# Gate logits made by token between output tiles, and a Sinkhorn iteration of five steps over five half groups

## The chip, the cores and the metric

The kernel runs on one core of a Trainium2 chip. The metric is the device time of one execution in microseconds (us), median of several runs. Before the change it is 1752.17 us (3 runs, 1752.05 to 1754.75).

## The reference

Three stages follow each other. All operands are float32.

```
p_packed = softmax(scale * p @ k.T) @ v            # 4 batches x 8 heads, 32 packed rows
a        = softmax(scale * q @ p_packed.T) @ p_packed   # 576 rows per batch and head
x        = a as [N = 2304 tokens, D = 512]
logits   = x @ w_gate                              # [N, E = 8]
P        = exp(logits - logits.max())              # one maximum over everything
8 times:  P /= P.sum(1) + 1e-9 ; P /= P.sum(0) + 1e-9 ; P *= N / E
x        = sum over e of P[:, e] * (relu(x @ w1[e]) @ w2[e])    # F = 1024
h        = relu(x @ w_in)                          # F = 2048
out      = (s * h * h + b) @ w_out
```

Each product of the experts and of the last stage is made of three passes over high and low parts (hi x hi, hi x lo, lo x hi), in a float32 type that TensorE runs in one pass.

## The kernel before, in words

The kernel is written by hand, one instruction stream per engine, with semaphores between them; nothing reorders it. TensorE (`pe`) multiplies, ScalarE (`act`) copies and exponentiates, VectorE (`dve`) makes the low parts, adds outputs and does the Sinkhorn steps, GpSimd (`pool`) splits weights and products into high and low parts, SyncE issues loads.

Since a is a product of the small attention weights `a` (here `a_hi`, `a_lo`, in the tensor `a_parts`: 2 quads of heads x 2304 tokens) and of the packed values, the kernel never forms x. It multiplies the packed values with the weights first (`packed_products`, `packed_gates`; results `g_parts` and, for the gate, `gw_both` and `gw_high`), and then with `a`.

The experts are 32 groups (8 experts x 4 parts of 256 hidden columns). A group has two half groups (u = 0, 1), each of 9 tiles of 128 tokens. A half group is written (g,u) below. On TensorE a half group is: four `hidden` calls (12 matmuls of 288 columns each; results in PSUM banks 2 to 5), between them two calls of `packed_products` for the next group, then nine output tiles (`outputs`, 6 matmuls of 512 columns each, PSUM banks 0 and 1 in turn). VectorE makes `h_lo` four times, then adds each output tile to `acc` (lines 1013 to 1021). Tile t on TensorE waits until VectorE has taken tile t-2. ScalarE makes `h_hi` and copies products to `g_raw`, which GpSimd splits (lines 557 and 559) as it does the weights (lines 534 to 551).

The gate: behind the outputs of half group (0,0), `gate_logits` makes logits by expert. The stationary side is `gw_both` (16 useful columns in 128: 8 of the high part, 8 of the low part, the rest zeros that GpSimd's memsets wrote) or `gw_high`, and the tokens move, 288 at a time: 8 spans x 2 quads x 2 = 32 matmuls. ScalarE copies each span (16 rows) to `logitsT`, which lies in the `acc` tensor. After two `hidden` calls, `turn_logits` turns it into tokens by expert with 18 transposes, and VectorE reads them (`logits_by_token`), finds the maximum, and the exponential follows in half group (1,0).

Sinkhorn: VectorE takes a step behind some of the output tiles (`sinkhorn`, line 1037). In each of the half groups (1,0), (1,1), (2,0), (2,1) two iterations are done, their steps behind tiles 0 to 4 and 5 to 8: sums and inverses of the rows, product by row, column part, column inverses (which needs a matmul with `ones` on TensorE behind the same tile, result in bank 7), product by column. The second iteration of a half group does its last two steps behind tile 8. Groups 1 to 3 add unscaled outputs; the finished gate is needed when `acc` is scaled, behind half group (3,1).

All matmuls have line 1221 (transposes have lines 1241, 1425 and 1455), the helper that records them, so they are told apart by tensors: `PS<-a_parts,gw_both` are the logits, `PS<-a_parts,g_parts` the hidden matmuls, `PS<-w_hi,h_hi` (and the two like it) the outputs, `PS<-w_hi,pp_parts` the packed products, `PS<-col_sum,ones` the column sums, which as float32 are two passes each.

Of the kernel before, what the change touches and what calls it, by code (L numbers as in the profile page):

```python
# [5 lines left out]
F32 = mybir.dt.float32  # L6
# [12 lines left out]
def attention_moe_mlp(nc, q, k, v, p, w_gate, w1, w2, w_in, w_out, s_, b_, out):  # L19
# [36 lines left out]
    with ExitStack() as ctx:  # L56
# [36 lines left out]
        gw_both = sb("gw_both", [P, QUADS, B, P], F32R)  # L93
        gw_high = sb("gw_high", [P, QUADS, B, P], F32R)
# [60 lines left out]
        logitsT = scratch[0:2 * E, UT * DM:UT * DM + N]  # L155
# [4 lines left out]
        LAST_TR, LAST_S2B = (5, 4, 3), (4, 6, 4)  # L160

        GWB, LG, LGT = 7, (2, 3, 4, 5), 0
# [29 lines left out]
        wg_ready = sem("wg_ready")  # L192
# [3 lines left out]
        lg_copied = sem("lg_copied")  # L196
        lgT_full = sem("lgT_full")
# [34 lines left out]
        SINKHORN_UNITS = [(1, 0), (1, 1), (2, 0), (2, 1)]  # L232
        COLUMN_SUMS = [(g, u, t) for g, u in SINKHORN_UNITS for t in (3, UT - 1)]
        assert len(COLUMN_SUMS) == SINKHORN_ITERATIONS
        UNSCALED = PER_EXPERT
        FIRST = UNSCALED + 1

# [284 lines left out]
        def _(pool):  # L522
# [4 lines left out]
            nc.gpsimd.memset(gw_both[:].bitcast(F32), 0.0).then_inc(wg_ready, 1)  # L527
            nc.gpsimd.memset(gw_high[:].bitcast(F32), 0.0).then_inc(wg_ready, 1)
# [86 lines left out]
        def _(act):  # L615
# [252 lines left out]
        def _(dve):  # L868
# [104 lines left out]
            def row_inverses():  # L973
                link(nc.vector.tensor_reduce(row_sum[:], gate[:], AX.X, ALU.add))
                link(nc.vector.tensor_scalar(row_sum[:], row_sum[:], EPS, None, ALU.add))
                link(nc.vector.reciprocal(row_inverse[:], row_sum[:]))  # L976

            def rows_divided():
                link(nc.vector.tensor_tensor(gate[:], gate[:], row_inverse[:].unsqueeze(2).to_broadcast([P, TILES, E]),  # L979
                                             ALU.mult))  # L980
# [737 lines left out]
```

## Time and profile before

| | before |
|---|---|
| median of 3 runs | 1752.17 us (1752.05 to 1754.75) |
| profiled execution | 1751.18 us |
| its span | 1749.4 us |
| PE (TensorE matmul) busy | 1739.2 us, 99% |
| PEld (TensorE weight load) busy | 1516.6 us, 87% |
| DVE (VectorE) busy | 916.5 us, 52% |
| ACT (ScalarE) busy | 710.0 us, 41% |
| POOL (GpSimd) busy | 609.1 us, 35% |

The span runs from the first to the last instruction; the time of an execution is 1.8 us more. Matmuls overlap: a listed duration holds the way through the array, so the pace of a stream is read from start to start. Busy time of an engine that is not waited for costs nothing.

### The profile page before, as it was taken

How to read it: one execution, taken by the hardware profiler on the slowest of the kernel's cores; microseconds unless marked ns; L12 is line 12 of the kernel's file. 1: busy time of each engine (PE TensorE's matmuls, PEld its weight loads, DVE VectorE, ACT ScalarE, POOL GpSimd, SP SyncE). 2: the span in 40 equal slices, each digit the busy share in tenths (PEclk: the TensorE clock that was granted, in tenths of full speed). 3: DMA queues.
4: the chain of work that ended last, by engine and by line, in shares of the span. 5: the costliest groups of instructions: out<-in, count | busy, mean ns of one | idle time of the engine just before them, and what ended most of it. 6: DMA issues, size and time to landing. Idle time of an engine off the chain costs nothing.

```text
span 1749.4 us, 27331 instructions
## 1 busy us (share of the span) xinstructions
PE 1739.2 (99%) x10257; PEld 1516.6 (87%) x10257; DVE 916.5 (52%) x1371; ACT 710.0 (41%) x1564; POOL 609.1 (35%) x380
## 2 busy tenths in 40 slices
PE   9999999999999999999999999999999999999999
PEld 7888888898889888888889888988888888888887
DVE  4846645445544445445544454455446555555555
ACT  5544465344434443444344443444343222222222
POOL 1263334434444344444444344344441001111100
PEclk9999999999999999999999999999999999999999
DMA  9431111111211111111211111112000000000002
GB/s 282 119 74 44 40 37 37 37 37 36 58 38 36 48 36 36 36 36 45 51 36 48 36 36 36 36 36 58 26 24 25 13 25 25 25 24 24 0 0 108
DMA packets 71776, 78.81 MB, mean 45 GB/s; under 512 B 7984, under 2 KB 59184, under 8 KB 71728
## 3 DMA queue, kind: packets, MB, share of 16 engines
q1 hardware_dynamic: 71728, 78.15, 16.6%
q8 instruction: 33, 0.54, 0.1%
q14 instruction: 15, 0.12, 0.0%
HBM read 73.42 MB, written 4.72 MB: 45 GB/s over the span
## 4 chain that ended last, share of the span: by engine, by line
PE 97%; DVE 1%; SPq 1%; DMA 0%; ACT 0%; issue 0%; DVEq 0%
PE PS L1221 95%; PE PS L1241 1%; DVE acc L1016 1%; DMA k_raw<-k_dram 0%; PE PS L1455 0%; DVE gate L993 0%; SPq L413 0%; ACT g_raw L617 0%; DVE gate L979 0%; SPq L437 0%; SPq L430 0%; SPq L418 0%; PE PS L1425 0%; DVE col_sum L983 0%; DVE row_inverse L976 0%
## 5 line engine op out<-in xcount | busy, mean ns | idle before, releaser
L1221 PE MATMUL PS<-w_hi,h_hi 128*128 128x512 f32 x1440 | 563.5, 391 | 1.3 <-DVE acc L1016 1.3
L1221 PE MATMUL PS<-w_hi,h_lo 128*128 128x512 f32 x1440 | 561.0, 390 | 0.0
L1221 PE MATMUL PS<-w_lo,h_hi 128*128 128x512 f32 x1440 | 560.8, 389 | 0.0
L1021 DVE SCALAR_TENSOR_TENSOR acc<-PS,gate,acc 128x512 f32<-128x512 f32 x504 | 377.8, 750 | 267.1 <-PE PS L1221 267.1
L694 ACT ACTIVATE h_hi<-PS 128x576 fp32r<-128x576 f32 x256 | 167.0, 653 | 675.1 <-PE PS L1221 674.4
L1221 PE MATMUL PS<-a_parts,g_parts 128*128 128x288 f32 x3072 | 438.1, 295 | 0.0
L1221 PEld LDWEIGHTS PS<-a_parts,g_parts 128*128 128x128 f32 x3072 | 419.3, 188 | 5.3 <-issue 0.4
L617 ACT ACTIVATE g_raw<-PS 32x256 f32<-32x256 f32 x992 | 373.1, 376 | 14.5 <-PE PS L1221 0.4
L1002 DVE SCALAR_TENSOR_TENSOR h_lo<-PS,h_hi 128x576 fp32r<-128x576 f32 x256 | 193.8, 757 | 323.5 <-ACT h_hi L694 323.4
L1221 PEld LDWEIGHTS PS<-w_hi,h_hi 128*128 128x128 f32 x1440 | 270.4, 188 | 57.7 <-DVE acc L1016 3.8
L1221 PEld LDWEIGHTS PS<-w_hi,h_lo 128*128 128x128 f32 x1440 | 270.3, 188 | 57.4
L1221 PEld LDWEIGHTS PS<-w_lo,h_hi 128*128 128x128 f32 x1440 | 270.4, 188 | 52.4
L534 POOL CAST w_hi<-stage 128x1024 fp32r<-128x1024 f32 (+1 forms) x78 | 76.8, 984 | 381.1 <-PE PS L1221 375.0
L557 POOL CAST g_parts<-g_raw 128x1024 fp32r<-128x1024 f32 x62 | 64.5, 1041 | 388.7 <-ACT g_raw L617 388.7
L536 POOL TENSOR_TENSOR w_lo<-stage,w_hi 128x1024 fp32r<-128x1024 f32 (+1 forms) x78 | 169.9, 2178 | 6.2
L1016 DVE TENSOR_TENSOR acc<-PS,acc 128x512 f32<-128x512 f32 x180 | 124.1, 689 | 54.1 <-PE PS L1221 53.4
L559 POOL TENSOR_TENSOR g_parts<-g_raw,g_parts 128x1024 fp32r<-128x1024 f32 x62 | 148.7, 2399 | 5.0
L852 ACT ACTIVATE mlp_f<-PS 128x512 f32<-128x512 f32 (+1 forms) x80 | 44.5, 556 | 220.0 <-PE PS L1221 220.0
L1221 PE MATMUL PS<-a_parts,w_hi 128*128 128x512 f32 (+1 forms) x320 | 117.8, 368 | 0.0
L1221 PE MATMUL PS<-a_parts,w_lo 128*128 128x512 f32 (+1 forms) x320 | 117.7, 368 | 0.0
L1221 PE MATMUL PS<-g_parts,w_hi 128*128 128x512 f32 (+1 forms) x320 | 117.7, 368 | 0.0
L1190 DVE SCALAR_TENSOR_TENSOR mlp_f<-mlp_f,s_and_b 128x512 f32<-128x512 f32 (+1 forms) x80 | 58.6, 733 | 100.4 <-ACT mlp_f L852 100.3
(131 smaller groups left out, 1051.8 us busy)
## 6 DMA issues: line engine op xcount, KB each, us to landing
stage<-moe_w_dram SPq DMA_DIRECT2D x96, 512.0 KB, 4.8
k_raw<-k_dram SPq DMA_DIRECT2D x8, 512.0 KB, 6.1
q_raw<-q_dram SPq DMA_DIRECT2D x8, 512.0 KB, 6.0
v_raw<-v_dram SPq DMA_DIRECT2D x8, 512.0 KB, 6.1
stage<-moe_w_in_dram SPq DMA_DIRECT2D x16, 256.0 KB, 2.8
stage<-moe_w_out_dram SPq DMA_DIRECT2D x8, 512.0 KB, 3.2
out_dram<-acc SPq DMA_DIRECT2D x16, 256.0 KB, 2.2
p_twice<-p_dram SPq DMA_DIRECT2D x8, 64.0 KB, 4.8
```

What stands on the lines that cost most here:

```text
L534: nc.gpsimd.tensor_copy(hi, src).then_inc(w1_ready, 1)
L536: nc.gpsimd.tensor_tensor(lo, src, hi.bitcast(F32), ALU.subtract).then_inc(w1_ready, 1)
L557: nc.gpsimd.tensor_copy(g_hi[par][:, Q], g_raw[Q][:]).then_inc(g_hi_ready, 1)
L559: nc.gpsimd.tensor_tensor(g_lo[par][:, Q], g_raw[Q][:], g_hi[par][:, Q].bitcast(F32), ALU.subtract).then_inc(g_lo_ready, 1)
L617: return nc.scalar.activation(dst, src, ACT.Copy)
L694: nc.scalar.activation(dst.rearrange("p (i n) -> p i n", i=2), src, ACT.Relu).then_inc(h_hi_ready, 1)
L852: nc.scalar.activation(mlp_f[:, slot, f, 0:n], bank(HB + 2 * slot + f, n), ACT.Relu).then_inc(relu_ready, 1)
L1002: nc.vector.scalar_tensor_tensor(out=h_lo[:, f, cols].rearrange("p (i n) -> p i n", i=2), in0=bank(HB + 2 * f, 2 * BANK).rearrange("p (i n ...
L1016: return nc.vector.tensor_tensor(dst, y, dst, ALU.add)
L1021: return nc.vector.scalar_tensor_tensor(out=dst, in0=y, scalar=share, in1=dst, op0=ALU.mult, op1=ALU.add)
L1190: nc.vector.scalar_tensor_tensor(out=r, in0=r, scalar=s_and_b[:, 0:1], in1=r, op0=ALU.mult, op1=ALU.mult).then_inc(f_ready, 1)
L1221: return nc.tensor.matmul(dst, lhsT, rhs, start=start, stop=stop)
```

## The change

There are two parts. Lines in the changed kernel are a few higher.

First, the logits are made by token. The tokens become the stationary side, 128 at a time, and `gw_both` (16 columns) or `gw_high` (8 columns) moves. The result of a tile of 128 tokens lands as [128 tokens, 16] in PSUM bank 5. A tile that lies in two batches (tiles 4 and 13) is done twice, with the gate of either batch, and VectorE takes the lower 64 rows from the second one. The matmuls stand between output tiles 4 to 8 of half group (0,0), three tiles of tokens (for tile 8: one) behind each output tile, and the last five tiles of tokens behind tile 8. The copies to `logitsT`, the transposes and the memsets are gone. The last transposes of the attention use bank 2 in place of 5, `hidden(0, 1, 0, 1)` waits until VectorE has read the logits, and a call of `packed_products` moves ahead of it.

Second, a Sinkhorn iteration is always five steps behind five successive tiles, and the eight iterations are spread over the half groups (1,0) to (3,0) by a list of starts. The reciprocal of the row sums moves from the first step to the second.

```
-        gw_both = sb("gw_both", [P, QUADS, B, P], F32R)
-        gw_high = sb("gw_high", [P, QUADS, B, P], F32R)
+        gw_both = sb("gw_both", [P, QUADS, B, 2 * E], F32R)
+        gw_high = sb("gw_high", [P, QUADS, B, 2 * E], F32R)
...
-        LAST_TR, LAST_S2B = (5, 4, 3), (4, 6, 4)
-        GWB, LG, LGT = 7, (2, 3, 4, 5), 0
+        LAST_TR, LAST_S2B = (2, 4, 3), (4, 6, 4)
+        GWB, LGB = 7, 5
+        HALVED = [t for t in range(TILES) if t * P // S != (t * P + P - 1) // S]
...
-        SINKHORN_UNITS = [(1, 0), (1, 1), (2, 0), (2, 1)]
-        COLUMN_SUMS = [(g, u, t) for g, u in SINKHORN_UNITS for t in (3, UT - 1)]
+        SINKHORN_UNITS = [(1, 0), (1, 1), (2, 0), (2, 1), (3, 0)]
+        SINKHORN_STARTS = [0, 5, 11, 17, 22, 27, 32, 37]
+        def sinkhorn_step(g, u, t):
+            if not isinstance(g, int) or (g, u) not in SINKHORN_UNITS:
+                return None
+            slot = SINKHORN_UNITS.index((g, u)) * UT + t
+            for i, first in enumerate(SINKHORN_STARTS):
+                if first <= slot < first + 5:
+                    return i, slot - first
+            return None
...
@ gpsimd
-            nc.gpsimd.memset(gw_both[:].bitcast(F32), 0.0).then_inc(wg_ready, 1)
-            nc.gpsimd.memset(gw_high[:].bitcast(F32), 0.0).then_inc(wg_ready, 1)
@ scalar
-            for n in range(2 * B):
-                act.wait_ge(lg_full, n + 1)
-                copy(logitsT[:, n * SPAN:(n + 1) * SPAN], bank(LG[n % 4], SPAN)[0:2 * E, :]
-                     ).then_inc(lg_copied, 1)
@ vector, logits_by_token
-                dve.wait_ge(lgT_full, 1)
-                by_token = bank(LGT)[:, 0:TILES * 2 * E].rearrange("p (t e) -> p t e", t=TILES)
+                dve.wait_ge(lg_full, 1)
+                both = bank(LGB)[:, 0:(TILES + len(HALVED)) * 2 * E].rearrange("p (t e) -> p t e", e=2 * E)
+                by_token, of_next = both[:, 0:TILES, :], both[HALF:P, TILES:TILES + len(HALVED), :]
                 link(nc.vector.tensor_copy(gate_part[:], by_token[:, :, E:2 * E]))
                 link(nc.vector.tensor_tensor(gate_part[:], by_token[:, :, 0:E], gate_part[:], ALU.add))
+                halves = gate_part[HALF:P, HALVED[0]:TILES:HALVED[1] - HALVED[0], :]
+                link(nc.vector.tensor_copy(halves, of_next[:, :, E:2 * E]))
+                link(nc.vector.tensor_tensor(halves, of_next[:, :, 0:E], halves, ALU.add))
@ vector, sinkhorn (steps 0 to 4 behind five successive tiles)
-                if t in (0, 5):
-                    row_inverses()
...
+                if step[1] == 0:
+                    row_sums()
+                if step[1] == 1:
+                    rows_divided()
+                if step[1] == 2:
+                    column_part()
+                if step[1] == 3:
+                    column_inverses(step[0])
+                if step[1] == 4:
+                    columns_divided(step[0])
@ vector: logits_by_token() moves ahead of lo_of_hidden(0, 1, 0, 0)
@ tensor
+            def gate_logits(tiles):
+                def tile(t, b, at):
+                    cols, cols_out = slice(t * P, (t + 1) * P), LGB * BANK + at * 2 * E
                     for Q in range(QUADS):
-                        mm(bank(LG[n % 4], SPAN), gw_both[:, Q, n // 2, :], a_hi[:, Q, cols], Q == 0, False)
-                        last = mm(bank(LG[n % 4], SPAN), gw_high[:, Q, n // 2, :], a_lo[:, Q, cols], False,
+                        mm(PS[:, cols_out:cols_out + 2 * E], a_hi[:, Q, cols], gw_both[:, Q, b, :], Q == 0, False)
+                        last = mm(PS[:, cols_out:cols_out + E], a_lo[:, Q, cols], gw_high[:, Q, b, 0:E], False,
                                   Q == QUADS - 1)
+                    return last
+                for t in tiles:
+                    last = tile(t, t * P // S, t)
+                    if t in HALVED:
+                        last = tile(t, t * P // S + 1, TILES + HALVED.index(t))
+                return last
...
@ tensor, behind output tile t of half group (0,0)
+                if t == 4:
+                    pe.wait_ge(gw_ready, 2 * B)
+                if t >= 4:
+                    gate_logits(range(3 * (t - 4), min(3 * (t - 3), HALVED[-1])))
...
-            gate_logits()
+            wait_evacuated(pe, [LAST + NC - 1])
+            gate_logits(range(HALVED[-1], TILES)).then_inc(lg_full, 1)
             pe.wait_ge(first_split, 4)
-            pe.wait_ge(lg_copied, 6)
             hidden(0, 1, 0, 0, weights(0, 1, 0, 0), (a_hi, a_lo))
-            pe.wait_ge(lg_copied, 8)
+            packed_products(1, 1, 0)
+            pe.wait_ge(top_part, 1)
             hidden(0, 1, 0, 1, weights(0, 1, 0, 1), (a_hi, a_lo))
-            turn_logits()
-            packed_products(1, 1, 0)
             hidden(0, 1, 1, 0, weights(0, 1, 1, 0), (a_hi, a_lo))
```

On TensorE, before, this is the end of the logits and what follows; 15 such pairs of rows stand ahead of it, and the last transposes are the turnings:

```order
L1221 MATMUL PS<-a_parts,gw_both 128x288
L1221 MATMUL PS<-a_parts,gw_high 128x288
L1221 MATMUL PS<-a_parts,g_parts 128x288 x24
L1425 MATMUL PS<-ident,acc 128x16 x18
L1221 MATMUL PS<-w_hi,pp_parts 128x256
L1221 MATMUL PS<-w_lo,pp_parts 128x256
```

On TensorE, in the changed kernel, at the same place, the end of the 14 pairs of rows behind output tile 8 of half group (0,0):

```order
L1232 MATMUL PS<-gw_both,a_parts 128x16
L1232 MATMUL PS<-gw_high,a_parts 128x8
L1232 MATMUL PS<-a_parts,g_parts 128x288 x12
L1232 MATMUL PS<-w_hi,pp_parts 128x256
L1232 MATMUL PS<-w_lo,pp_parts 128x256
L1232 MATMUL PS<-w_hi,pp_parts 128x256
L1232 MATMUL PS<-w_lo,pp_parts 128x256
L1232 MATMUL PS<-a_parts,g_parts 128x288 x24
```

The turnings are gone, the packed products stand after one hidden call instead of two, and the order of the names shows that tokens and gate weights have changed sides. 12, 16, 12, 12 and 28 such small matmuls stand behind output tiles 4, 5, 6, 7 and 8.

On VectorE, before, the second half group of Sinkhorn, (1,1), from its h_lo to tile 4 (`acc` is an output tile, the others are steps):

```order
L1002 SCALAR_TENSOR_TENSOR h_lo<-PS,h_hi 128x576 x4
L1016 TENSOR_TENSOR acc<-PS,acc 128x512
L974 TENSOR_REDUCE row_sum<-gate 128x18
L975 TENSOR_SCALAR row_sum<-row_sum 128x18
L976 RECIPROCAL row_inverse<-row_sum 128x18
L1016 TENSOR_TENSOR acc<-PS,acc 128x512
L979 TENSOR_TENSOR gate<-gate,row_inverse 128x144
L1016 TENSOR_TENSOR acc<-PS,acc 128x512
L983 TENSOR_REDUCE col_sum<-gate 128x8
L1016 TENSOR_TENSOR acc<-PS,acc 128x512
```

On VectorE, in the changed kernel, the same half group from its h_lo on:

```order
L1013 SCALAR_TENSOR_TENSOR h_lo<-PS,h_hi 128x576 x4
L1027 TENSOR_TENSOR acc<-PS,acc 128x512
L1004 TENSOR_TENSOR gate<-gate,col_sum 128x144
L1027 TENSOR_TENSOR acc<-PS,acc 128x512 x2
L985 TENSOR_REDUCE row_sum<-gate 128x18
L986 TENSOR_SCALAR row_sum<-row_sum 128x18
L1027 TENSOR_TENSOR acc<-PS,acc 128x512
L989 RECIPROCAL row_inverse<-row_sum 128x18
L990 TENSOR_TENSOR gate<-gate,row_inverse 128x144
L1027 TENSOR_TENSOR acc<-PS,acc 128x512
L994 TENSOR_REDUCE col_sum<-gate 128x8
L1027 TENSOR_TENSOR acc<-PS,acc 128x512
```

The half group now begins with the last step of the iteration before, has a tile without a step, and its own iteration starts behind tile 2.

## Rows read from the trace of the kernel before

**Rows 1.** The page: span, granted clock by slice, chain that ended last.
```profile
span 1749.4 us, 27331 instructions
...
PEclk9999999999999999999999999999999999999999
...
PE 97%; DVE 1%; SPq 1%; DMA 0%; ACT 0%; issue 0%; DVEq 0%
```

**Rows 2.** TensorE's waits: line, awaited, us in total, times, longest.
```profile
PE PS L1221 <- DVE col_sum L983: 1.6, 2, 0.8
PE PS L1221 <- DVE acc L1016: 1.3, 4, 0.6
```

**Rows 3.** Timeline of TensorE about the logits: start us, us, engine, line, operation.
```profile
99.18 0.29 PE L1221 MATMUL PS<-a_parts,gw_both 128*128 128x288 f32 x1
...
104.09 3.34 PE L1221 MATMUL PS<-a_parts,g_parts 128*128 128x288 f32 x24
107.36 1.29 PE L1425 MATMUL PS<-ident,acc 16*128 16x16 f32 x18
108.58 0.39 PE L1221 MATMUL PS<-w_hi,pp_parts 128*128 128x256 f32 x1
108.80 0.28 PE L1221 MATMUL PS<-w_lo,pp_parts 128*128 128x256 f32 x1
```

**Rows 4.** Timeline of VectorE: the first h_lo of seven successive half groups from (1,0).
```profile
128.30 0.76 DVE L1002 SCALAR_TENSOR_TENSOR h_lo<-PS,h_hi 128x576 fp32r<-128x576 f32 x1 [1.51 <-ACT h_hi L694]
...
150.50 0.76 DVE L1002 SCALAR_TENSOR_TENSOR h_lo<-PS,h_hi 128x576 fp32r<-128x576 f32 x1 [1.47 <-ACT h_hi L694]
...
171.35 0.76 DVE L1002 SCALAR_TENSOR_TENSOR h_lo<-PS,h_hi 128x576 fp32r<-128x576 f32 x1 [1.01 <-ACT h_hi L694]
...
193.19 0.76 DVE L1002 SCALAR_TENSOR_TENSOR h_lo<-PS,h_hi 128x576 fp32r<-128x576 f32 x1 [1.46 <-ACT h_hi L694]
...
213.92 0.76 DVE L1002 SCALAR_TENSOR_TENSOR h_lo<-PS,h_hi 128x576 fp32r<-128x576 f32 x1 [0.72 <-ACT h_hi L694]
...
233.47 0.76 DVE L1002 SCALAR_TENSOR_TENSOR h_lo<-PS,h_hi 128x576 fp32r<-128x576 f32 x1 [1.57 <-ACT h_hi L694]
...
253.03 0.76 DVE L1002 SCALAR_TENSOR_TENSOR h_lo<-PS,h_hi 128x576 fp32r<-128x576 f32 x1 [1.58 <-ACT h_hi L694]
```

**Rows 5.** TensorE's weight loads: two groups (busy us, mean ns), then timeline rows.
```profile
L1221 PEld LDWEIGHTS PS<-a_parts,gw_both 128*128 128x128 f32 x16 | 3.0, 188 | 0.7 <-ACT acc L617 0.6
L1425 PEld LDWEIGHTS PS<-ident,acc 16*128 16x128 f32 x18 | 1.2, 137 | 0.2 <-issue 0.2
...
107.36 1.19 PEld L1425 LDWEIGHTS PS<-ident,acc 16*128 16x128 f32 x18 [0.16 <-issue]
...
138.59 0.30 PEld L1221 LDWEIGHTS PS<-col_sum,ones 128*128 128x128 f32 x2 [0.24 <-DVE col_sum L983]
138.80 0.19 PEld L1221 LDWEIGHTS PS<-w_hi,h_hi 128*128 128x128 f32 x1
138.91 0.19 PEld L1221 LDWEIGHTS PS<-w_lo,h_hi 128*128 128x128 f32 x1
```

**Rows 6.** Timeline of TensorE's matmuls on both sides of a column sum.
```profile
138.38 0.39 PE L1221 MATMUL PS<-w_hi,h_lo 128*128 128x512 f32 x1
...
138.83 0.48 PE L1221 MATMUL PS<-w_hi,h_hi 128*128 128x512 f32 x1
```

**Rows 7.** Timelines of GpSimd and VectorE in half groups (1,1) and (2,0).
```profile
162.28 2.40 POOL L559 TENSOR_TENSOR g_parts<-g_raw,g_parts 128x1024 fp32r<-128x1024 f32 x1
...
183.08 2.40 POOL L559 TENSOR_TENSOR g_parts<-g_raw,g_parts 128x1024 fp32r<-128x1024 f32 x1
...
163.38 1.46 DVE L993 TENSOR_TENSOR gate<-gate,col_sum 128x144 f32<-128x144 f32 x1
...
170.03 0.31 DVE L993 TENSOR_TENSOR gate<-gate,col_sum 128x144 f32<-128x144 f32 x1
```

**Rows 8.** Timeline of TensorE: the second column sum of half group (1,0).
```profile
147.63 0.39 PE L1221 MATMUL PS<-col_sum,ones 128*128 128x8 f32 x2 [0.79 <-DVE col_sum L983]
```

More of the change, by code:

```diff
@@ L1037, in sinkhorn @@
             def sinkhorn(g, u, t):
-                if (g, u) not in SINKHORN_UNITS or t is None:
+                step = sinkhorn_step(g, u, t) if t is not None else None
+                if not step:
                     return
-                if (g, u, t) == (*SINKHORN_UNITS[0], 0):
+                if step == (0, 0):
                     dve.wait_ge(gate_exp, 1)
-                if t in (0, 5):
-                    row_inverses()
-                if t in (1, 6):
+                if step[1] == 0:
+                    row_sums()
+                if step[1] == 1:
                     rows_divided()
-                if t in (2, 7):
+                if step[1] == 2:
                     column_part()
-                if t in (3, 8):
-                    column_inverses(COLUMN_SUMS.index((g, u, t)))
-                if t in (4, 8):
-                    columns_divided(COLUMN_SUMS.index((g, u, 3 if t == 4 else 8)))
+                if step[1] == 3:
+                    column_inverses(step[0])
+                if step[1] == 4:
+                    columns_divided(step[0])
             def scaled_then_shared(dst, y, tile):
@@ L1072, in _ @@
             off_max2(0, 0)
-            dve.wait_ge(wg_ready, 2)
             gates_of_packed(0)
@@ L1141, in _ @@
                     a_chunk(last, t - 5)
+            logits_by_token()
             lo_of_hidden(0, 1, 0, 0)
             lo_of_hidden(0, 1, 0, 1)
-            logits_by_token()
             lo_of_hidden(0, 1, 1, 0)
@@ L1405, in packed_gates @@
                 last.then_inc(gw_full, 1)
-            def gate_logits():
-                pe.wait_ge(gw_ready, 2 * B)
-                for n in range(2 * B):
-                    if n == 1:
-                        wait_evacuated(pe, [LAST + NC - 1])
-                    if n >= 4:
-                        pe.wait_ge(lg_copied, n - 3)
-                    cols = slice(n * SPAN, (n + 1) * SPAN)
+            def gate_logits(tiles):
+                def tile(t, b, at):
+                    cols, cols_out = slice(t * P, (t + 1) * P), LGB * BANK + at * 2 * E
                     for Q in range(QUADS):
-                        mm(bank(LG[n % 4], SPAN), gw_both[:, Q, n // 2, :], a_hi[:, Q, cols], Q == 0, False)
-                        last = mm(bank(LG[n % 4], SPAN), gw_high[:, Q, n // 2, :], a_lo[:, Q, cols], False,
+                        mm(PS[:, cols_out:cols_out + 2 * E], a_hi[:, Q, cols], gw_both[:, Q, b, :], Q == 0, False)
+                        last = mm(PS[:, cols_out:cols_out + E], a_lo[:, Q, cols], gw_high[:, Q, b, 0:E], False,
                                   Q == QUADS - 1)
-                    last.then_inc(lg_full, 1)
-            def turn_logits():
-                pe.wait_ge(acc_done, UT)
-                for t in range(TILES):
-                    last = nc.tensor.transpose(bank(LGT)[:, t * 2 * E:(t + 1) * 2 * E],
-                                               logitsT[:, t * P:(t + 1) * P], ident[0:2 * E, 0:2 * E])
-                last.then_inc(lgT_full, 1)
+                    return last
[4 more added lines that the diff above has]
+                return last
             def spans(part, t, u, half):
@@ L1474, in outputs @@
                         between(t)
-                    if isinstance(g, int) and (g, u, t) in COLUMN_SUMS:
-                        i = COLUMN_SUMS.index((g, u, t))
+                    step = sinkhorn_step(g, u, t)
+                    if step and step[1] == 3:
+                        i = step[0]
                         pe.wait_ge(col_part, i + 1)
```

12 lines of the change are left out of this document (4 added, 8 removed).

## The prediction

> **What bounds the kernel now.** I read the page first. The span is 1749.4 us and the chain that ended last is TensorE for 97% of it [rows 1]. A microsecond of TensorE's queue is therefore a microsecond of the kernel, and work on another engine counts only where TensorE waits for it. Next the table of TensorE's waits: the largest are for VectorE, 1.6 us for the column sums and 1.3 us for output tiles [rows 2]; both lie in the Sinkhorn stretch. Then the timelines of the two places that the change touches.
>
> The logits (TensorE's timeline, [rows 3]): the first of 32 gate matmuls starts at 99.18 and the next hidden matmul at 104.09, so they hold the queue 4.91 us, a short wait for ScalarE's copies inside. The 24 hidden matmuls that follow are busy 3.34 us; about 0.295 of that is the length of one, so their spacing is (3.34 - 0.295) / 23 = 0.132, and what follows them could start at 104.09 + 24 x 0.132 = 107.27. It starts at 108.58 and lasts 0.39 where its equal lasts 0.28: the 18 turnings of the logits cost 1.31 + 0.1 = 1.4 us.
>
> The Sinkhorn stretch: the first h_lo of each half group [rows 4] gives the length of a half group. Undisturbed it is 253.03 - 233.47 = 19.56. The four that hold Sinkhorn take 22.20, 20.85, 21.84 and 20.73: excesses of 2.64, 1.29, 2.28 and 1.17, together 7.4 us. The fifth, from 213.92, takes 19.55 and is clean.
>
> **Part 1: the logits.** Removed: 4.91 + 1.4 = 6.3 us of TensorE's queue. Eight copies on ScalarE (16x288) go too; TensorE waited for them only inside the 4.91.
>
> Added: 18 tiles and two halves give 20 places, each with 2 quads x 2 matmuls = 80 matmuls. Columns streamed fall from 32 x 288 = 9216 to 40 x 16 + 40 x 8 = 960, but loads of a stationary side rise from 32 to 80, each of 128 columns of tokens, and 8 or 16 columns hide no load. So the price is that of a load. The nearest row is the column sum: it is two passes of an 8-column matmul, each behind a load of 128 columns. Its two loads start at 138.59, the next two (of the following output tile, whose type is that of the new matmuls) at 138.80 and 138.91 [rows 5]: three steps in 0.32, 0.107 each, where nothing but the loads sets the pace. One load is listed with 188 ns for either type [rows 5]. From the matmuls' side: the large one ahead of the column sum starts at 138.38, the one behind it is listed at 138.83 with 0.48 in place of 0.39 [rows 6], 0.32 for the two short ones, of which about 0.1 is the first load, issued late because it waited for VectorE. In the new stream no load waits. I take 0.107: 80 x 0.107 = 8.6 us. The lower end is the turnings: 18 loads of 16x128, busy 1.19 us with 137 ns for one, so (1.19 - 0.137) / 17 = 0.062 [rows 5]; they are transposes, and one of their loads is shorter (137 against 188), so they weigh little. The upper end is no overlap at all between one load and the next: 0.188. Over 80 matmuls the ends are 5.0 and 15.0 us.
>
> The Trainium skill ("TensorE: Matmul & The Clock Gate", section "Back-to-back issue gap") gives 81 ns for a sustained pair of load and 128-column matmul; by that rule the 80 would cost 6.5 us and the whole change come out 2 us under before. The same page's section "LDWEIGHTS (loading the stationary operand)" gives a load as its columns over 1.2 GHz, 107 ns here, and the rows agree with this one; no row shows the 81.
>
> Net of part 1: 8.6 - 6.3 = +2.3 us (ends -1.3 and +8.7).
>
> Where they stand costs nothing more: a tile's tokens are ready (batches 0 to 2 were split before output tile 0), VectorE and ScalarE gain time between outputs, and what is queued behind is the next tile alone. The packed products of group 1 come 12 matmuls later, 1.3 us, and with them ScalarE's copies of the products and GpSimd's split; all that waits for these moves later by more. After the last logit there is a new wait (the top of the logits, read from bank 5, before hidden (0,1,0,1)); behind it on TensorE's queue stands the rest of the hidden block. In front of it lie 12 hidden matmuls of 0.132 and four packed products of 0.117 (107 ns of columns and a little; [rows 3] has two of them, 0.28 long each), 2.1 us. VectorE needs in that time five operations: one over all 144 values undisturbed lasts 0.31 [rows 7]; five at 0.33 with their links are at most 1.65, and two of them are smaller. With 0.25 for the end of the last matmul that is 1.9 at most, 1.6 likely. No wait, with a margin of half a microsecond; if it is missed the price is well under 1 us.
>
> The two memsets that go from GpSimd's start lie beside loads that TensorE waits for, and their results are first used tens of microseconds later: 0.
>
> **Part 2: Sinkhorn over five half groups.** The eight column sums on TensorE stay, about 0.32 each [rows 6], 2.6 us. The rest of the excess, 7.4 - 2.6 = 4.8 us, is stall, the most that can be gained. A tile takes 6 matmuls, 1.36 us; TensorE's tile t+2 needs VectorE's output t, which takes 0.69 after whatever step stood ahead of it, so a single step up to about 1.2 us is free. Undisturbed, all five steps are below that (0.3 to 0.9). What makes the stalls are the products gate<-gate,col_sum and gate<-gate,row_inverse: 0.31 us at 170.03, but 1.46 at 163.38, ending just after GpSimd's 2.40 us operation that began at 162.28 [rows 7]. A product of two SBUF operands on VectorE waits until the GpSimd operation under way ends. So I place each new step against GpSimd's times:
> - (1,0): the same steps on the same tiles, except that the reciprocal moves one tile on and the last product goes to the next half group. Its two long products still end when GpSimd does, and the wait of 0.79 before the column sum at 147.63 [rows 8] stays. Gain 0.
> - (1,1): one whole iteration, tiles 2 to 6: rows' product at about 161.9 (in a 1.04 us cast, short wait), columns' product at about 166.0, after GpSimd's operation of 162.28 has ended. No stall, one column sum: 1.29 becomes 0.33. Gain 1.0.
> - (2,0): steps of two iterations. Rows' product on tile 0 (GpSimd idle), columns' product on tile 3 at about 182.7 (ends before the operation at 183.08 [rows 7] or just in it), rows' product on tile 5 at about 185.8 (waits to about 186.6 and fits), column sum on tile 7 nearly in time, product on tile 8 free. 2.28 becomes two sums and 0.2. Gain 1.4.
> - (2,1): tiles 0 to 8 as before. Gain 0.1.
> - (3,0), so far clean: one column sum and about 0.1. Loss 0.4.
> Together 2.1 us gained; ends 0 (the collisions only move) and 4.8.
>
> The Trainium skill ("GPSIMD Engine Reference", section "8. Key points") says that GpSimd shares its SBUF interfaces with VectorE, contending with operations of two SBUF inputs. By the rule the cost depends on where a step meets GpSimd; if only the number of steps in a half group mattered, the gain would be nearer 4.8. The rows are on the rule's side (1.46 against 0.31).
>
> **Sum.** +2.3 - 2.1 = +0.2 us. The profiled execution took 1751.2 us (span 1749.4 and 1.8 around it), so 1751.4 on its scale; the median of the runs, 1752.2, lies 1.0 above it. I give 1752.4.
>
> **Rivals.**
> 1. Loads are cheap. If the short matmuls follow at 0.062 as the turnings do, part 1 is -1.3, and with 2.1 from Sinkhorn the time is 1748.8; with all stalls gone (4.8) it is 1746.1. For it: the turnings' row. Against: the three steps of 0.107. Chance 0.13.
> 2. Halfway between these rows, 0.085 a pair: 6.8 us, so +0.5 - 2.1 and 1750.6. Chance 0.10. (The page's 81 ns would stand here.)
> 3. Slower: no load overlaps with a short matmul in front of it that adds to the same PSUM columns, so that each pair takes a load's whole 0.188. 15.0 us, +8.7 - 2.1, 1758.8. Its place is the 28 small matmuls behind tile 8 and the four groups ahead; it decides from 0.15 a pair ((3.5 + 2.1 + 6.3) / 80). For it: such a long stream stands nowhere in the trace; against: the column sum's two passes add to the same columns at 0.107. Chance 0.12.
> 4. The Sinkhorn part doesn't do what it says: the new places meet GpSimd as often. Gain 0, time 1754.5. For it: two of the four half groups are unchanged; against: (1,1) and (2,0) hold less. Chance 0.08.
> The clock is no rival of weight: the granted clock is at its upper level in every slice, those with many small transposes included [rows 1].
>
> **Numbers.** The forecast has 0.57; its own range is 1750.3 to 1754.8. What this kernel's measurement can tell is 0.2%, 3.5 us: 1748.7 and 1755.7. Faster: rival 1 for the most part and the forecast's edge, 0.16. Slower: rival 3 and edges of 4 and the forecast, 0.14. Same 0.70. The range of 8 in 10 takes in rivals 2, 4 and the near part of 1, and some of the way to 3: 1748.2 to 1756.8.
>
> **What would show it.** In the new trace the loads of a_parts with gw_both as moving side start 0.107 apart, and the block behind tile 8 is 28 x 0.107 = 3.0 us long; 0.06 or 0.19 there proves rival 1 or 3. TensorE has no idle time before hidden (0,1,0,1). Half groups: about 22.2, 19.9, 20.4, 20.7, 20.0. If the first is shorter by more than 0.3 us, my reading that GpSimd's end sets those products is wrong; if the second or third is not shorter, the placing against GpSimd is.

## Result and the profile after

| | before | after |
|---|---|---|
| median of 20 runs each, in turns | 1752.11 us (1750.77 to 1758.42) | 1754.63 us (1752.66 to 1759.39) |
| ratio | | 1.0013, 95% interval 1.0007 to 1.0019 |
| profiled execution, span | 1751.18, 1749.4 us | 1755.19, 1753.4 us |
| mean granted clock of it | 1.000 | 0.999 |

The changed kernel is slower by 2.3 us (1.2 to 3.3), within the 0.2% that was called no change. Forecast was 1752.4 with a range of 1748.2 to 1756.8.

The page of after, to set beside [rows 1]:

```profile
span 1753.4 us, 27385 instructions
...
PE 1742.6 (99%) x10287; PEld 1520.7 (87%) x10287; DVE 915.4 (52%) x1373; ACT 706.1 (40%) x1556; POOL 606.6 (35%) x378
...
PEclk9999999999999999999999999999999999999999
...
PE 98%; DVE 1%; DMA 0%; ACT 0%; issue 0%; SPq 0%; DVEq 0%
```

TensorE sets the end as before. Each digit of the clock row stands for 44 us and hides what a narrower view shows further down.

TensorE's waits for VectorE in after (line, awaited, us in total, times, longest), against [rows 2]:

```profile
PE PS L1252 <- DMA k_tail<-k_dram: 1.7, 1, 1.7
...
PE PS L1232 <- DVE col_sum L994: 0.9, 1, 0.9
PE PS L1232 <- DVE acc L1027: 0.8, 2, 0.6
```

The waits for VectorE fell from 2.9 to 1.7 us. The wait for `k_tail`, a load at the very start, was 0.4 us in the profile of before; it changes from profile to profile and does not belong to the change (last experiments).

The ledger of the comparison is made of the starts of one instruction, the first `hidden` matmul of a half group. For (0,0), whose first two `hidden` calls stand a few us earlier, it is the first matmul of the last two calls. In after, on TensorE (start us, us; the first row is half group (0,0), the others (1,0) to (4,0)):

```profile
82.38 3.44 PE L1232 MATMUL PS<-a_parts,g_parts 128*128 128x288 f32 x24
...
131.04 0.29 PE L1232 MATMUL PS<-a_parts,g_parts 128*128 128x288 f32 x1
...
153.08 0.38 PE L1232 MATMUL PS<-a_parts,g_parts 128*128 128x288 f32 x1
...
173.17 0.29 PE L1232 MATMUL PS<-a_parts,g_parts 128*128 128x288 f32 x1
...
193.93 0.29 PE L1232 MATMUL PS<-a_parts,g_parts 128*128 128x288 f32 x1
...
214.63 0.38 PE L1232 MATMUL PS<-a_parts,g_parts 128*128 128x288 f32 x1
...
235.20 0.29 PE L1232 MATMUL PS<-a_parts,g_parts 128*128 128x288 f32 x1
...
254.76 0.29 PE L1232 MATMUL PS<-a_parts,g_parts 128*128 128x288 f32 x1
```

In before they stand at 81.19, 125.83, 147.88, 168.73, 190.57, 211.36, 231.00 and 250.56; the first two in TensorE's timeline:

```profile
81.19 3.44 PE L1221 MATMUL PS<-a_parts,g_parts 128*128 128x288 f32 x24
...
125.83 3.35 PE L1221 MATMUL PS<-a_parts,g_parts 128*128 128x288 f32 x24
```

The differences from each start to the next:

| us | (0,0)+(0,1), logits | (1,0) | (1,1) | (2,0) | (2,1) | (3,0) | (3,1) |
|---|---|---|---|---|---|---|---|
| before | 44.64 | 22.05 | 20.85 | 21.84 | 20.79 | 19.64 | 19.56 |
| after | 48.66 | 22.04 | 20.09 | 20.76 | 20.70 | 20.57 | 19.56 |
| change | +4.02 | 0.0 | -0.76 | -1.08 | -0.09 | +0.93 | 0 |
| forecast | +2.3 | 0 | -1.0 | -1.4 | -0.1 | +0.4 | |

So the logits cost 4.0 us in place of 2.3, and Sinkhorn gives 1.0 in place of 2.1. To these net 3.0 us comes the start of (0,0), 1.19 us later; behind (3,1) the changed kernel wins back 0.2, and the spans differ by 4.0.

**The logits.** The block behind tile 8 and what follows, TensorE's timeline of after (start us, us), against [rows 3]:

```profile
106.13 0.17 PE L1232 MATMUL PS<-gw_both,a_parts 128*128 128x16 f32 x1
106.15 0.25 PE L1232 MATMUL PS<-gw_high,a_parts 128*128 128x8 f32 x1
...
109.06 0.25 PE L1232 MATMUL PS<-gw_high,a_parts 128*128 128x8 f32 x1
109.17 2.71 PE L1232 MATMUL PS<-a_parts,g_parts 128*128 128x288 f32 x12
111.68 0.41 PE L1232 MATMUL PS<-w_hi,pp_parts 128*128 128x256 f32 x1
...
112.53 3.64 PE L1232 MATMUL PS<-a_parts,g_parts 128*128 128x288 f32 x24
```

28 small matmuls take 109.17 - 106.13 = 3.04 us, and from the second to the last they stand (109.06 - 106.15) / 26 = 0.112 us apart. The price was read right from [rows 5], 0.107. What comes behind was not foreseen: twelve hidden matmuls take 2.51 us where 12 x 0.132 = 1.58 was due, and four packed products take 0.85 for 0.47, with 0.41 in place of 0.28 listed for one. TensorE waits for nothing there. The granted clock of these stretches tells why (us, then busy time and count of PE, PEld, DVE, ACT and POOL, then PEclk, DMA share, GB/s):

```profile
106.00:108.00 2.00, 2.00 (x20) 1.96 (x18) 0.69 (x1) 0.00 (x0) 1.92 (x2) 1.00 0.00 0
...
109.00:110.00 1.00, 1.00 (x9) 1.00 (x9) 0.61 (x2) 0.00 (x0) 1.00 (x2) 0.90 0.00 0
110.00:111.00 1.00, 1.00 (x6) 1.00 (x6) 0.66 (x3) 0.00 (x0) 0.92 (x2) 0.50 0.00 0
111.00:112.00 1.00, 1.00 (x6) 1.00 (x6) 0.00 (x0) 0.09 (x1) 1.00 (x1) 0.50 0.00 0
112.00:113.00 1.00, 1.00 (x6) 1.00 (x6) 0.40 (x1) 0.56 (x1) 0.68 (x1) 0.50 0.00 0
113.00:114.00 1.00, 1.00 (x8) 1.00 (x8) 0.35 (x1) 0.00 (x0) 0.00 (x0) 0.90 0.00 0
```

Behind the block the clock stands at its lower level (0.50, 1.2 of 2.4 GHz) from about 109.8 to 113.1, some 3.3 us, while TensorE is busy without a gap, as it is from 96 us on (13.00 of 13.00 us up to 109). The cost is 0.93 + 0.38 + 0.30 (the 24 hidden matmuls: 3.64 for 3.34) = 1.6 us.

The new wait for the top of the logits costs nothing, as said. VectorE in after, its last operation for the logits:

```profile
110.46 0.30 DVE L982 TENSOR_REDUCE top<-gate_part 128x1 f32<-128x144 f32 x1
```

It ends at 110.76; the matmul that waits for it begins at 112.53, and without the fall of the clock it would have begun at 109.17 + 1.58 + 0.47 = 111.22, still behind it.

**Sinkhorn.** VectorE in after, two products in (1,0), one in (1,1), then a step in (2,0) and one in (3,0), against [rows 7]:

```profile
146.39 1.78 DVE L1004 TENSOR_TENSOR gate<-gate,col_sum 128x144 f32<-128x144 f32 x1
...
150.25 1.49 DVE L990 TENSOR_TENSOR gate<-gate,row_inverse 128x144 f32<-128x144 f32 x1
...
162.81 0.30 DVE L1004 TENSOR_TENSOR gate<-gate,col_sum 128x144 f32<-128x144 f32 x1
...
188.89 0.98 DVE L986 TENSOR_SCALAR row_sum<-row_sum 128x18 f32<-128x18 f32 x1
...
230.26 1.30 DVE L1001 TENSOR_SCALAR col_sum<-col_sum 128x8 f32<-128x8 f32 x1
```

GpSimd's operations of more than 2 us beside them:

```profile
145.60 2.41 POOL L570 TENSOR_TENSOR g_parts<-g_raw,g_parts 128x1024 fp32r<-128x1024 f32 x1
...
149.15 2.42 POOL L547 TENSOR_TENSOR w_lo<-stage,w_hi 128x1024 fp32r<-128x1024 f32 x1
...
187.44 2.39 POOL L570 TENSOR_TENSOR g_parts<-g_raw,g_parts 128x1024 fp32r<-128x1024 f32 x1
...
229.14 2.39 POOL L570 TENSOR_TENSOR g_parts<-g_raw,g_parts 128x1024 fp32r<-128x1024 f32 x1
```

The products of two SBUF operands end when GpSimd's operation does: 148.17 with 148.01, 151.74 with 151.57. In (1,0) both long ones are still there and still make TensorE wait, 0.56 us for a tile at 148.95 and 0.87 for the column sum at 152.83, to set beside [rows 8]. But two operations on 8 and 18 columns, with one tensor operand, wait in the same way: 0.98 us (ends 189.87; GpSimd 189.83) and 1.30 (231.56; 231.53), where undisturbed ones last 0.17. Neither was counted in the forecast. Each makes an output tile of VectorE late, and TensorE's next tile but one with it, by some 0.35 us with the load behind it (at 190.64 and 232.34).

### The profile page after: what moved, and what is told of

The parts are those of the page before. It is cut to its first block, busy times and chain, and to the rows that moved or that the text cites. A ratio compares the mean times of both kernels' runs of the same rounds, so it can differ in the third digit from the quotient of the medians.

```text
span 1753.4 us, 27385 instructions
## 1 busy us (share of the span) xinstructions
PE 1742.6 (99%) x10287; PEld 1520.7 (87%) x10287; DVE 915.4 (52%) x1373; ACT 706.1 (40%) x1556; POOL 606.6 (35%) x378
## 4 chain that ended last, share of the span: by engine, by line
PE 98%; DVE 1%; DMA 0%; ACT 0%; issue 0%; SPq 0%; DVEq 0%
PE PS L1232 96%; PE PS L1252 2%; PE PS L1461 0%; DVE acc L1027 0%; DMA k_raw<-k_dram 0%; DVE gate L1004 0%; ACT acc L658 0%; DVE gate L990 0%; DVE col_sum L1001 0%; DVE row_sum L986 0%; SPq L450 0%; DVE stat L897 0%; ACT acc L628 0%; SPq L431 0%; SPq L426 0%
```

## The experiments

For each kernel n is its number of runs. The mean granted clock of an execution tells whether the clock fell in it: 3.3 us at half the rate are 3.3 x 0.5 / 1753 = 0.0009, so 1.000 becomes 0.999. It does not tell where the clock fell, and a fall of less than some 1.7 us is rounded away (1.7 x 0.5 / 1753 = 0.0005). The figures "at 1.000" are medians over executions with that mean clock. The first four kernels stand against a before of 1751.83 us that was timed beside them (35 runs, 30 of them at 1.000: 1751.74).

**The logits alone.** The changed kernel with the Sinkhorn part of before.

```
-        SINKHORN_UNITS = [(1, 0), (1, 1), (2, 0), (2, 1), (3, 0)]
-        SINKHORN_STARTS = [0, 5, 11, 17, 22, 27, 32, 37]
+        SINKHORN_UNITS = [(1, 0), (1, 1), (2, 0), (2, 1)]
+        COLUMN_SUMS = [(g, u, t) for g, u in SINKHORN_UNITS for t in (3, UT - 1)]
```

> The new logits with the Sinkhorn placing of the kernel before. Theory (the loss is the 80 loads, 8.9 us for 6.3, and 1.6 us of half clock that follows the block of 28 small matmuls): against before +4.0 us in TensorE's ledger, from the hidden block of half group (0,0) to that of (1,0) 48.7 us for 44.6, granted clock 0.50 in about 3 us behind the block, and about 1755.5 to 1756.5 as median. Rival (the clock's fall is a chance of one profiled execution): no fall here, ledger +2.6, median about 1754.7.

Measured: 1755.30 us (n 11), ratio 1.0020 (1.0011 to 1.0029). The stretch of the logits takes 48.74 us, the half groups 22.04, 20.82, 21.89, 20.91 and 19.65 as in before. Three executions at 1.000 have 1754.11, seven at 0.999 have 1755.80. So the logits alone cost 3.5 us, and the clock's part goes with them: at 1.000 they cost 1754.11 - 1751.74 = 2.4. The profiled execution has the clock at 0.50 at the same place as after, from 109.7 to 113.1 us.

**Sinkhorn alone.** The kernel before with the Sinkhorn part of after (the opposite of the diff above).

> The new Sinkhorn placing with the logits of the kernel before. Theory (Sinkhorn gives back 1.0 us: (1,1) 0.8 and (2,0) 1.1 shorter, (3,0) 0.9 longer): five half groups from (1,0) on 104.2 us for 105.2, no fall of the clock, median 1.0 below before, about 1751.1. Rival (the prediction's placing, 2.1 us): 1750.0. Rival (it only moves stalls): 1752.1.

Measured: 1750.74 us (n 12), ratio 0.9998 (0.9990 to 1.0007); 11 executions at 1.000, median 1750.70. Half groups 22.06, 20.09, 20.79, 20.70 and 20.38: 104.02 in place of 105.17, a gain of 1.15 us. The interval of the ratio takes in 1, so the gain rests on these starts and on the medians at 1.000 (1750.70 against 1751.74). By medians it is -1.1; with the logits alone (+3.5) this makes +2.4, and the medians of the whole change differ by 2.5. The parts add up.

**Blocks of 16.** The same 80 small matmuls, 16 behind each of tiles 4 to 8, instead of 12, 16, 12, 12 and 28. My theory was that only the long block lets the clock fall.

```
-                if t >= 4:
-                    gate_logits(range(3 * (t - 4), min(3 * (t - 3), HALVED[-1])))
+                if 4 <= t < 8:
+                    gate_logits([(0, 1, 2, 3), (4, 5, 6), (7, 8, 9, 10), (11, 12, 14, 15)][t - 4])
...
-            gate_logits(range(HALVED[-1], TILES)).then_inc(lg_full, 1)
+            gate_logits([13, 16, 17]).then_inc(lg_full, 1)
```

> The changed kernel, its 80 small matmuls in five blocks of 16 (tiles 0 to 3; 4 to 6; 7 to 10; 11, 12, 14, 15; 13, 16, 17 behind output tiles 4 to 8) in place of 12, 16, 12, 12, 28. Theory (the fall of the clock comes from the 28 in a row): granted clock stays at its upper level, 1.6 us less than the changed kernel, about 1753.0. Rival (the fall comes from the share of small matmuls in the whole stretch from output tile 4 on, whatever their blocks): the clock falls as before and the time is the changed kernel's, 1754.6.

Measured: 1754.21 us (n 12), ratio 1.0020 (1.0009 to 1.0031). Seven executions at 1.000 (median 1753.22), five below it, down to two at 0.995 (1760.51 and 1761.07). The profiled one is among the five; TensorE's timeline in it:

```profile
102.10 0.48 PE L1232 MATMUL PS<-w_hi,h_hi 128*128 128x512 f32 x1
...
104.09 0.36 PE L1232 MATMUL PS<-gw_both,a_parts 128*128 128x16 f32 x1
...
108.08 0.63 PE L1232 MATMUL PS<-w_hi,h_lo 128*128 128x512 f32 x1
108.50 0.63 PE L1232 MATMUL PS<-w_hi,h_hi 128*128 128x512 f32 x1
```

The clock fell here among large matmuls, behind a block of 16, and stayed at 0.50 from 103.4 to about 110 (the small ones 0.21 apart, the large ones 0.42). My theory fell: without the block of 28 the clock still falls. Mean clocks below 1.000 are rarer than with the block of 28 (5 of 12 against 24 of 31) but four of the five are lower than 0.999, so the falls are longer where they come. The rival, that the share of small matmuls in the whole stretch decides, is not borne out as it was put either (it gave the changed kernel's 1754.6 and falls as before, and seven of 12 executions have none to be seen); what decides is not shown.

**Half the loads.** The changed kernel without the 40 matmuls of `gw_high` with the tokens' low parts; the low parts of the attention weights are missing from its logits.

```
-                        mm(PS[:, cols_out:cols_out + 2 * E], a_hi[:, Q, cols], gw_both[:, Q, b, :], Q == 0, False)
-                        last = mm(PS[:, cols_out:cols_out + E], a_lo[:, Q, cols], gw_high[:, Q, b, 0:E], False,
+                        last = mm(PS[:, cols_out:cols_out + 2 * E], a_hi[:, Q, cols], gw_both[:, Q, b, :], Q == 0,
```

> The changed kernel without the matmuls of the low parts of the attention weights in the logits (that part of the logits is left out): 40 small matmuls in place of 80, blocks of 6, 8, 6, 6, 14. Theory (each small matmul costs its load, 0.111 us, and the clock falls only after a long block): 4.4 us less and no fall, 1.6 us less again, 6.0 together, about 1748.6. Rival (the price is per block and wait, not per load): less than 3 us less.

Measured: 1748.59 us (n 11), ratio 0.9982 (0.9974 to 0.9991), ten of 11 at 1.000. The stretch of the logits takes 42.77 us; what is removed (6.32) and 40 loads of 0.111 give 44.64 - 6.32 + 4.44 = 42.76. The price per load is confirmed, and with half of them the clock stays up in ten of 11 executions (their blocks are half as long too, 14 at most).

**Sinkhorn steps clear of GpSimd.** The logits of before; the five steps of an iteration are given tiles one by one, so that none meets an operation of GpSimd that would hold it past the slack, over six half groups (slot = 9 x half group + tile).

```
+        SINKHORN_UNITS = [(1, 0), (1, 1), (2, 0), (2, 1), (3, 0), (3, 1)]
+        STEP_TILES = [(0, 1, 2, 3, 8), (8, 9, 10, 11, 14), (14, 15, 16, 17, 18), (18, 19, 20, 21, 26),
+                      (26, 27, 28, 29, 32), (32, 33, 34, 35, 36), (36, 37, 38, 39, 44), (44, 45, 46, 47, 48)]
```

> The logits of the kernel before; the 40 Sinkhorn steps placed by a table over six half groups, so that no product and no scaling of VectorE falls behind a tile in which GpSimd works for long (first four steps of an iteration behind tiles 0 to 3 or 6 to 8, the last with the next iteration's first behind tile 8 or 5). Theory (the stalls come from SBUF products that wait for GpSimd, so clear places have none): only the eight column sums at 0.32 are left, 2.7 us in place of 7.4, no gate product over 0.6 us, TensorE idle for none of them; against before -4.6 us, median about 1747.3. Rival (any Sinkhorn step costs TensorE something wherever it stands; spreading gives no more than the change's): -1.0 to -2.0, about 1750.3.

Measured (before, timed beside this and the next three kernels: 1751.61, 22 runs, 19 at 1.000): 1747.48 us (n 11), ratio 0.9980 (0.9971 to 0.9989); nine at 1.000, median 1747.07. Half groups 19.95, 20.16, 20.09, 20.17, 20.12 and 19.95: above 19.56 they hold 3.1 us in all, hardly more than the eight column sums (2.6). Two groups of VectorE's table tell what changed (count, then busy us and mean ns of one), first after:

```profile
L1004 DVE TENSOR_TENSOR gate<-gate,col_sum 128x144 f32<-128x144 f32 x8 | 5.2, 656 | 0.0
L990 DVE TENSOR_TENSOR gate<-gate,row_inverse 128x144 f32<-128x144 f32 x8 | 3.8, 469 | 0.3
...
L1001 DVE TENSOR_SCALAR col_sum<-col_sum 128x8 f32<-128x8 f32 x8 | 3.0, 369 | 0.3
```

and then with the steps clear of GpSimd:

```profile
L987 DVE TENSOR_TENSOR gate<-gate,row_inverse 128x144 f32<-128x144 f32 x8 | 2.5, 309 | 0.3
L1001 DVE TENSOR_TENSOR gate<-gate,col_sum 128x144 f32<-128x144 f32 x8 | 2.4, 305 | 0.0
```

All sixteen products now last 0.31 us, and TensorE has no wait for VectorE's steps or tiles left. The steps are also spread over one half group more than in the change, but the products' length shows that what went is the wait for GpSimd. By medians 4.1 us could be had (1.9 to 5.1 by the ratio), and the change took 1.1: its five successive tiles leave little freedom to step around GpSimd.

**Small among large.** The changed kernel with its 80 small matmuls in 20 groups of four, spread among the large matmuls of tiles 4 to 8.

```
-                    gate_logits(range(3 * (t - 4), min(3 * (t - 3), HALVED[-1])))
...
+                        if behind:
+                            behind()       # gate_place: 4 small ones behind large matmul 2, 3, 5 and 6
```

> The changed kernel with its 80 small matmuls in 20 groups of four between the large matmuls of output tiles 4 to 8, so that none stands in a long block. Theory (the clock falls when small matmuls stand in long blocks): the granted clock stays up in all executions, ledger from the hidden block of (0,0) to that of (1,0) about 47.3, median about 1753.2 with little scatter. Rival (what counts is the share of small matmuls in some microseconds, as in blocks of 16): the clock falls in a part of the executions, for several us when it does, and the scatter is that of the blocks of 16 (up to 1761).

Measured: 1753.16 us (n 11), ratio 1.0010 (1.0001 to 1.0019); nine of 11 at 1.000, median 1752.93 against 1751.59 for before. In the profiled one the clock is 1.00 in the whole stretch of the logits, which takes 46.99 us, +2.35. That is the forecast's +2.3, with no fall of the clock in it. With the same number of loads, where they stand decides the other 1.6 us.

The mean clock of this execution is 0.999 all the same. The fall stands at another place, from 10.4 to 13.7 us, among the transposes and small products of the first stage, long before the gate:

```profile
9.00:10.00 1.00, 0.55 (x4) 0.42 (x4) 0.00 (x0) 0.56 (x3) 0.00 (x0) 1.00 1.13 236
10.00:11.00 1.00, 1.00 (x17) 0.20 (x16) 0.00 (x0) 0.60 (x1) 0.00 (x0) 0.58 1.15 332
```

So my expectation that the clock stays up in every execution missed, but the one fall that can be placed has nothing to do with the gate's matmuls. Such falls come in kernels without them too: before has 11 of its 78 executions below 1.000.

**Clear of GpSimd, and copies first.** The kernel with the clear steps, and ScalarE copies the gate's logits ahead of the last five copies of products, for which the gate matmuls had waited.

```
-            shift_products(1, 0, range(4, SHIFTS))
+            shift_products(1, 0, range(4, 11))
...
+            shift_products(1, 0, range(11, SHIFTS))
```

> As the kernel with clear Sinkhorn places, and ScalarE copies the logits ahead of its last five product copies. Theory (in the kernel before, TensorE's 4.91 us of gate matmuls hold 0.6 us of waiting for ScalarE's copies): from the first gate matmul to the next hidden one 4.3 us, 0.5 us less in all, about 1746.8. Rival (the five copies then hold up relu, and the half microsecond comes back): the same as without.

Measured: 1746.21 us (n 6), ratio 0.9971 (0.9959 to 0.9983), the fastest of all: 5.1 us below before by the ratio. The 32 gate matmuls, in before 4.91 us, in this one:

```profile
99.32 0.29 PE L1229 MATMUL PS<-a_parts,gw_both 128*128 128x288 f32 x1
...
103.55 3.34 PE L1229 MATMUL PS<-a_parts,g_parts 128*128 128x288 f32 x24
```

4.23 us: 32 x 0.132, and no wait left in them, 0.7 less than before (0.5 was expected). Of the 6.3 us that the change removed, 0.7 could be had without moving the logits.

**One block of 80.** All small matmuls behind tile 8. A longer stream should make the fall of the clock certain, and show what small matmuls cost at the lower level.

```
-                if t >= 4:
-                    gate_logits(range(3 * (t - 4), min(3 * (t - 3), HALVED[-1])))
...
-            gate_logits(range(HALVED[-1], TILES)).then_inc(lg_full, 1)
+            gate_logits(range(TILES)).then_inc(lg_full, 1)
```

> The changed kernel with all 80 small matmuls in one block behind output tile 8. Theory (a long block of small matmuls makes the clock fall, and the longer the surer): the clock is at half in every execution, from within the block on, a load is then 0.213 apart instead of 0.111; mean clock 0.998 or less in all runs, median some 4 us or more above the changed kernel, about 1759. Rival (the fall is a matter of chance for any arrangement): clock and time scatter as in the changed kernel, median about 1754.6.

Measured: 1761.42 us (n 5), ratio 1.0048 (1.0034 to 1.0062); the clock fell in all five (0.995 to 0.997). The stretch of the logits takes 55.52 us, 10.9 more than before. TensorE's timeline where the clock falls, 2 us into the block that began at 99.89, and where the block ends:

```profile
101.93 0.25 PE L1232 MATMUL PS<-gw_high,a_parts 128*128 128x8 f32 x1
102.04 0.30 PE L1232 MATMUL PS<-gw_both,a_parts 128*128 128x16 f32 x1
102.19 0.36 PE L1232 MATMUL PS<-gw_high,a_parts 128*128 128x8 f32 x1
102.41 0.36 PE L1232 MATMUL PS<-gw_both,a_parts 128*128 128x16 f32 x1
...
114.78 3.23 PE L1232 MATMUL PS<-a_parts,g_parts 128*128 128x288 f32 x12
```

The spacing goes from 0.111 to 0.213 in the middle of a uniform stream in which nothing waits. The clock stays down from 102.1 to 119.2 us; 17.1 us at half the rate cost 8.5, and with the 2.4 of the loads that is the 10.9. TensorE is busy 10.00 of 10.00 us at a clock of 0.50:

```profile
104.00:114.00 10.00, 10.00 (x49) 10.00 (x48) 0.00 (x0) 0.00 (x0) 5.06 (x3) 0.50 0.17 50
```

**Memsets back.** The changed kernel with the wide gate tensors of before and GpSimd's two memsets at the start, to see whether the 1.19 us later start in (0,0) comes from their absence or from the tensors' places.

```
-        gw_both = sb("gw_both", [P, QUADS, B, 2 * E], F32R)
+        gw_both = sb("gw_both", [P, QUADS, B, P], F32R)
...
+            nc.gpsimd.memset(gw_both[:].bitcast(F32), 0.0).then_inc(wg_ready, 1)
```

> The changed kernel with the wide gate tensors, their memsets on GpSimd and so the memory layout of the kernel before; only 16 or 8 of 128 columns are used. Theory (the memsets and the layout cost nothing either way): the same as the changed kernel in the same call, within 0.5 us. Rival (the later start of TensorE's first hidden block in the changed kernel's profile, 82.4 us for 81.2, comes from the missing memsets or the layout): first hidden block back at 81.2 and the median 1 us below the changed kernel's.

**The changed kernel again,** beside it.

> The changed kernel itself, for its scatter. Theory (the clock falls in most executions): mean granted clock below 1.000 in more than half of them, and those with 1.000 about 1.5 us shorter than those with 0.999; median about 1754.5. Rival (the fall is rare and the profile was unlucky): most at 1.000.

Measured (before, timed beside both: 1751.56, 21 runs, 18 at 1.000): with memsets 1754.27 us (n 11), ratio 1.0008 (0.9998 to 1.0017); without, 1754.53 (n 11), ratio 1.0014 (1.0005 to 1.0023). Their profiles have the first row of the ledger at 81.43 and 81.35 (after: 82.38; before: 81.19), and the stretch of the logits at 48.69 and 48.68. TensorE's wait for `k_tail` is 1.7 us in after, 0.4 in before and absent in these two. So the later start was scatter of the first loads, the memsets and the layout cost nothing that can be seen, and the +4.0 of the logits repeats, with the clock at 0.50 from 109.4 to 112.9 in both.

Over the 31 executions of the changed kernel (20 and 11): seven at 1.000, median 1752.67; 17 at 0.999, median 1754.53; seven lower. Where the clock does not fall, the change costs about 1.1 us against the 1751.6 of before. Logits alone and memsets back, which have the same block of 28, are below 1.000 in eight of 11 each, so it is 40 of 53 in all.

## Why the prediction was right or wrong

**Right.** The time lies in the range, and "same" was the likeliest outcome. TensorE's queue is what counts; the price of a small matmul is that of its load, 0.111 us where 0.107 was read from three steps of one column sum. Rivals 1 to 3 (0.062, 0.085, 0.188) are gone: the spacing, and the kernel with half the loads, allow none of them. The removed 6.3 us are right to a tenth. The new wait for the logits' top, the later packed products and the missing memsets cost nothing. The stalls of Sinkhorn come from products that wait for GpSimd, shown by the kernel that avoids them; the first half group stays as it was (22.04 for 22.05).

**Luck.** That the time lies in the range is in part luck. It is 2.2 us above the forecast, and both large misses, the clock's 1.6 and Sinkhorn's 1.1, go the same way. The range reaches so far up for rivals 3 and 4, and neither is what happened. Rival 4's 1754.5 is nearly the measured 1754.63, but by a sum with no gain from Sinkhorn and no fall of the clock.

**Wrong: "The clock is no rival of weight".** The step reasoned from the row of the clock in [rows 1], where the kernel before is at its upper level in every slice although it has many small transposes. It had no stream like the new one, and a row with slices of 44 us would not show 3.3 us at half rate anyway; after's is the same. The sum had no term for it. The fall costs 1.6 us in the profile and 1754.53 - 1752.67 = 1.9 between the executions with and without it, more than any other miss. The runs show that it comes with the blocks of small matmuls: below 1.000 are 40 of 53 executions with the block of 28, five of five with all in one block, but one of 11 with half of them and two of 11 with them spread in fours, no more than before itself (11 of 78). All four profiled executions with the block of 28 have the fall behind it, 0.6 to 1.3 us after its last small matmul.

The Trainium skill ("TensorE: Matmul & The Clock Gate", section "HAM oscillation — how this bites in real kernels") puts such falls down to gaps in which TensorE is idle. The measurement differs here: in the block of 80 the clock fell with TensorE busy all the time from 96 us on, so the measurement decides.

**Wrong in size: Sinkhorn, -2.1 forecast, -1.0 and -1.15 measured.** Three terms of the sum:
- (1,1): -0.76 for -1.0. It holds 0.53 above 19.56, of which the column sum is 0.3; the rest lies in no wait that the trace shows.
- (2,0): -1.08 for -1.4. An operation I had counted as free of GpSimd, the addition of a constant to the row sums, waited 0.98 us (188.89), and TensorE's tile started 0.35 us late.
- (3,0): +0.93 for +0.4. The scaling of the column sums lasted 1.30 us in place of 0.17 (230.26), and TensorE's tile started 0.35 us late (with the load behind it) on its account. The column sum itself is 0.3; what remains, 0.3, lies in no wait that the trace shows (0.2 of it ahead of the first output tile, which comes 7.57 us behind the half group's start for 7.38 in before).

The rule read from [rows 7], that products of two SBUF operands wait for GpSimd, holds but was too narrow. Rival 4, no gain at all, is not borne out either: the five half groups of Sinkhorn take 104.2, 104.0 and 104.3 us in three profiles that hold the new part (after, Sinkhorn alone, the changed kernel again), against 105.2 before.

**The sum, corrected:** +2.4 for the loads, +1.6 to 1.9 for the clock in most executions, -1.1 for Sinkhorn gives +2.9 to 3.2 in an execution with a fall and +1.3 without; with about three of four executions falling, some +2.6. Measured +2.3 by the ratio (1.2 to 3.3) and +2.5 by the medians.

What stays open is what the chip looks at when it lowers the clock. The runs show which streams bring a fall more often, not a bound, and within one kernel it differs from execution to execution. Most falls are known only from the mean clock of an execution, which gives no place.

## What to carry to other kernels

Counting columns says nothing where the moving side has 8 or 16: there the number of loads is the price, 0.11 us each, and exchanging the sides of a product turned 32 matmuls of 0.132 into 80 of 0.111. Read the granted clock in windows of a microsecond around any new stream of short matmuls, compare executions by their mean clock, find the place of a fall in the trace before you blame a stream for it, and spread such matmuls among large ones if they must be there. A small step on VectorE should be placed against the times of GpSimd's long operations, not at equal distances; that alone was worth 4 us here, where the five successive tiles of the change got 1.1.

## What the runs showed of the hardware

- The clock fell to 1.2 GHz while TensorE was busy without a gap, behind or inside streams of small matmuls whose pace the loads set. The mean granted clock was below 1.000 in 40 of 53 executions with a block of 28, in 5 of 5 with one of 80, in 5 of 12 with blocks of 16, and in 11 of 78 of the kernel before.
- A load follows the granted clock: 0.111 us apart at the upper level, 0.213 at the lower. The Trainium skill ("TensorE: Matmul & The Clock Gate", section "LDWEIGHTS (loading the stationary operand)") gives columns over 1.2 GHz, 107 ns; the trace agrees at the upper level only.
- A fall can also stand far from the gate's matmuls: in the profile of the small ones among large at 10.4 to 13.7 us, with TensorE idle for 0.45 of the microsecond from 9 to 10. Idle time alone does not bring it: in after TensorE is busy 6.51 of the first 10.00 us, and the clock stays up.
- On VectorE also operations with one tensor operand in SBUF wait for GpSimd's operation to end (128x8: 1.30 us in place of 0.17; 128x18: 0.98 in place of 0.18).
- The same hidden matmul of (0,0) stood at 82.38 us in one profile of the changed kernel and at 81.35 in another: starts differ by a microsecond with the first loads, so parts of two profiles are better compared by differences of starts than by times from the beginning.
